# Moving an output copy one step later on ScalarE and the denominators' small term to GpSimd in an attention and expert kernel

## The chip, the cores and the metric
The kernel runs on one core of a Trainium2 chip. The metric is the device time of one execution in microseconds (us). Five engines work beside each other: TensorE (PE, with its weight loads shown as PEld), VectorE (DVE), ScalarE (ACT), GpSimd (POOL) and SyncE (SP, which issues DMAs). They meet through semaphores alone: an instruction increments one when it is done, another waits until it has reached a value.

## The reference
Attention over 2 x 8 heads of 768 positions with 64 dimensions. A query sees only the keys whose six projection signs are the same as its own:

```python
mask = q_bucket[:, :, :, None] == k_bucket[:, :, None, :]
scores = np.where(mask, scale * q @ k.T, -1e9)
scores = scores - np.max(scores, axis=-1, keepdims=True)
attn = np.exp(scores)
attn = attn / (np.sum(attn, axis=-1, keepdims=True) + 1e-09)
attn_out = attn @ v
```

Behind it stand a gated feed-forward layer over the 1536 rows and a layer of 8 experts that sends each row to one of them.

## The kernel before
**Pairs, steps and groups.** The 16 heads are worked as 8 pairs, P = 0 to 7. A pair has 12 steps j; each step takes 128 queries of one head against all 768 keys. Three steps make a group g, so a pair has four groups. A period is one pair's 12 steps. Periods 1 to 4 run in a hardware loop of two passes, the others are written out, with constant semaphore values. Period 8 has no scores of its own and drains what is left, beside the first units of the next layer.

**One step on the engines.** TensorE makes the scores of step j (L941, L942) into one of two banks ps_s. VectorE takes the maximum of each row, negated (L1609). ScalarE takes the exponentials with their sums psums (L1323, an ACTIVATE and a short read of the accumulator). When a group's three steps are done, VectorE adds 1e-9 to the three sums (L1621, denom) and takes the reciprocals (L1623, rden); GpSimd multiplies the three tiles of probabilities by them (L745, the normalization, which also adds alone, a term for rows that see no key, made on GpSimd at L734). The code calls this `denoms(P, g)` on VectorE and `put_alone(P, g)` on GpSimd.

**LAG = 5 steps later** TensorE transposes the normalized tiles, two blocks of keys in a step (L956), ScalarE copies each block to a high part in fp32r (L1333, `highs`), and VectorE subtracts to get the low part (L1629, `lows`). One step after that, TensorE multiplies both parts with v (L971, L973). Once a group's six blocks are summed, ScalarE copies the lower half of the output bank to SBUF (L1338, `half_out`) and VectorE adds the upper half to it (L1635, `x_out`), which frees the bank.

**The order of the work** is written out by hand in each engine's `period`. ScalarE before: highs(j), exps(j), then, at j = 2, 5, 8, 11, half_out. VectorE: max(j), at j = 0, 3, 6, 9 the denominators of the group before, lows(j), at the same j x_out, and at j = 1, 4, 7, 10 a comparison that makes bits for the next pair (L1584, L1586). GpSimd: alone of group g, then the three normalizations of group g, then a slot of other work: splitting q, k and v of later pairs into high and low parts (L630, L634, L650, L671), in periods 5 and 6 also squares for the next layer's norm (L701, L705), in period 7 low parts and weights for that layer (L716, L719, L762). `wait_apart` is GpSimd's wait; inside the loop it also increments a semaphore of its own.

In period 0, j = 3, ScalarE does one of the normalizations itself (L1399). At j = 0 of periods 1 to 5 it scales the queries of a later pair (L1318). In period 7 it makes high parts for the next layer (L1360) at the steps named in HIGHS_BESIDE_EXPS.

**What needs what around the change.** rden needs denom, and lows(j) stands behind rden in VectorE's queue. The normalization of a group needs rden and alone. The transposes of a group need its three normalizations, two steps later. x_out needs half_out.

Of the kernel before, what the change touches and what calls it, by code (L numbers as in the profile page):

```python
# [13 lines left out]
ALU = mybir.AluOpType  # L14
# [4 lines left out]
LAG = 5  # L19
# [7 lines left out]
def wait(eng, sem, value):  # L27

    if isinstance(value, int) and value <= 0:
        return  # L30
    eng.wait_ge(sem, value)


def build(nc, q, k, v, proj, w_gate, w_val, w_out, rms_g, router, out_gate, w1, w2, out):
# [17 lines left out]
    TG = N // G  # L52
    NT = N // P128
    E, _, FE = w1.shape
    CF = FE // P128

# [26 lines left out]
    with ExitStack() as ctx:  # L83
        addr = [nc.sbuf_base + 64]

        def at(name, shape, dt, offset=None):
            size = 4 if dt != BF16 else 2
            for n in shape[1:]:
                size *= n
            if offset is None:  # L90
                offset = addr[0] = (addr[0] + 31) // 32 * 32
                addr[0] += size
            return nc.alloc_sbuf_tensor_at(name, shape, dt, offset=offset)
# [4 lines left out]
        def sem(name):  # L98
            return ctx.enter_context(nc.semaphore(name))
# [81 lines left out]
        psums = at("psums", [P128, PRING], F32)  # L181
        denom = at("denom", [P128, PRING], F32)
# [88 lines left out]
        for i in range(3):  # L271
# [12 lines left out]
        ps_o = psum("ps_o", [P128, 512], F32)  # L284
        ps_p = psum("ps_p", [P128, 512], F32)

        names = ("first_low proj_places q_own proj_in const_set ident_ready proj_split proj_ready proj_ready_second prefilled "
                 "cleared blocks_set blocks_ready scales_ready first_high second_low ahead_high q_scaled qk_high qk_low v_split proj_made bits_ready scores_ready max_done "
                 "alone_put first_norm exp_done denom_done rden_ready norm_done turned high_ready low_ready pv_done "
                 "half_ready x_done pool_passed "  # L290
# [4 lines left out]
                 "hidT_high hidT_low "  # L295
                 "down_made outs_ready").split()
        sems = {n: sem(n) for n in names}
        (first_low, proj_places, q_own, proj_in, const_set, ident_ready, proj_split, proj_ready, proj_ready_second, prefilled, 
         cleared, blocks_set, blocks_ready, scales_ready, first_high, second_low, ahead_high, q_scaled, qk_high, qk_low, v_split, proj_made, bits_ready, scores_ready, max_done,
         alone_put, first_norm, exp_done, denom_done, rden_ready, norm_done, turned, high_ready, low_ready, pv_done,  # L300
         half_ready, x_done, pool_passed,
# [26 lines left out]
        def cols_of(tg):  # L328
            return slice((tg % 2) * G, (tg % 2 + 1) * G)
# [25 lines left out]
        def steps_of(P, j, lag):  # L355

            back = (j - lag) % PAIR_STEPS
            return (P if j >= lag else P - 1), back // 3, back % 3
# [58 lines left out]
        SQUARES_01 = 12  # L417
        LATE_LOWS = {0: slice(0, 2), 1: slice(2, 4), 2: slice(4, 5), 3: slice(5, 6), 4: slice(6, 8)}
        EARLY = {0: 2, 1: 6, 2: 2, 3: 2, 4: 2, 5: 2}
        HIGHS_BESIDE_EXPS = {1: 0, 3: 1, 5: 2, 7: 3, 10: 4}  # L420
        HIGHS_IN_TAIL = {0: (5,), 1: (6, 7)}

        def high_of(tg, c):
# [196 lines left out]
        def _(pool):  # L620
            def wait_apart(sem, value):

                wait(pool, sem, value)
                if not isinstance(value, int):
                    pool.sem_inc(pool_passed, 1)
# [101 lines left out]
            def put_alone(P, g):  # L727
                c = slice(3 * g, 3 * g + 3)

                wait_apart(norm_done, 12 * (P - 1) + 3 * g + 3)  # L730
                wait_apart(max_done, 12 * P + 3 * g + 3)
                if not (isinstance(P, int) and P == 0):
                    pool.wait_ge(first_norm, 1)
                nc.gpsimd.tensor_scalar(alone[:, c], negmax[:, c], MASKED, 1.0 / S,  # L734
                                        ALU.is_ge, ALU.mult).then_inc(alone_put, 1)
                wait_apart(alone_put, 4 * P + g + 1)

            def period(P, slots):
                for g in range(4):
                    put_alone(P, g)  # L740
                    wait_apart(rden_ready, 4 * P + g + 1)
                    own = 2 if isinstance(P, int) and P == g == 0 else 3
                    for j in range(3 * g, 3 * g + own):
                        pr = probs[:, j]
                        nc.gpsimd.tensor_scalar(pr, pr, rden[:, j:j + 1], alone[:, j:j + 1],  # L745
                                                ALU.mult, ALU.add).then_inc(norm_done, 4 - own if j % 3 == 1 else 1)
                    for steps, n in slots[g]:
                        some(n, steps)
# [89 lines left out]
            with pool.Fori(0, 2) as i:  # L838
                P = 2 * i + 1
# [452 lines left out]
        def _(act):  # L1292
# [28 lines left out]
            def exps(P, j):  # L1321
                wait(act, max_done, 12 * P + j + 1)
                nc.scalar.activation(probs[:, j].rearrange("p (a n) -> p a n", a=2), third(ps_s[j % 2]), ACT.Exp,  # L1323
                                     bias=negmax[:, j:j + 1],
                                     accum_out=psums[:, j:j + 1]).then_inc(exp_done, 1)

            def highs(P, g, jj):
                for kt in (2 * jj, 2 * jj + 1):
                    u = 6 * g + kt
                    wait(act, turned, 24 * P + u + 1)  # L1330

                    wait(act, pv_done, 24 * P + u - 3)
                    nc.scalar.activation(pT_h[u % 4][:], ps_t[kt % 2][:, 0:G], ACT.Copy).then_inc(high_ready, 1)  # L1333

            def half_out(P, g):
                wait(act, pv_done, 24 * P + 6 * (g + 1))
                wait(act, x_done, 4 * P + g)
                nc.scalar.activation(o_half[D:2 * D, :], value_banks[g % 2][D:2 * D, 0:G], ACT.Copy).then_inc(half_ready, 1)  # L1338
# [19 lines left out]
            def high_xn(b, c, cols=slice(0, S)):  # L1358

                nc.scalar.activation(xn[:, b, 0, c, cols], xT[:, C * b + c, cols], ACT.Copy,  # L1360
                                     scale=gain[:, c:c + 1]).then_inc(xnh_made, 1)
# [7 lines left out]
            def period(P, par, before=True, s=True, ahead=True):  # L1369
                for j in range(PAIR_STEPS):  # L1370
                    Pt, g, jj = steps_of(P, j, LAG)
                    if (j >= LAG and s) or (j < LAG and before):
                        highs(Pt, g, jj)
                    if s:
                        exps(P, j)
                    Pv, g, jj = steps_of(P, j, LAG + 1)
                    if jj == 2 and ((j >= LAG + 1 and s) or (j < LAG + 1 and before)):
                        half_out(Pv, g)
                    if s and not ahead and j in HIGHS_BESIDE_EXPS:
                        if j == 1:  # L1380
                            act.wait_ge(gates_in, 48)
                            act.wait_ge(scores_ready, PAIR_STEPS * LAST_PAIR)
                        tg, c = divmod(HIGHS_BESIDE_EXPS[j], C)
                        high_xn(0, c, cols_of(tg))
                    if not s and j in HIGHS_IN_TAIL:
                        for n in HIGHS_IN_TAIL[j]:
                            tg, c = divmod(n, C)
                            high_xn(0, c, cols_of(tg))
                    if not s and j in (1, 2, 3):
                        high_xn(1, j - 1)  # L1390
                    if not s and j == 0:
                        root((0, 1))
                    if not s and j == 4:
                        high_last(0)
                    if isinstance(P, int) and P == 0:
                        if j == 3:
                            act.wait_ge(rden_ready, 1)
                            act.wait_ge(alone_put, 1)
                            nc.scalar.activation(probs[:, 2], probs[:, 2], ACT.Identity, bias=alone[:, 2:3],  # L1399
                                                 scale=rden[:, 2:3]).then_inc(first_norm, 1)  # L1400
                        if j in (0, 3, 4):
                            high_ahead(1, 1, max(0, j - 2))
                        if j in (7, 8, 9):
                            high_ahead(2, 0, j - 7)
                    elif j == 0 and (not isinstance(P, int) or P <= LAST_PAIR - 2):
                        scale_queries(P + 2, par)
# [14 lines left out]
            with act.Fori(0, 2) as i:  # L1421
                P = 2 * i + 1
# [157 lines left out]
        def _(dve):  # L1580
# [31 lines left out]
            def denoms(P, g):  # L1612

                n = 4 * P + g + 1
                c = slice(3 * g, 3 * g + 3)

                wait(dve, norm_done, 3 * (n - 4))
                if not (isinstance(P, int) and P == 0):
                    dve.wait_ge(first_norm, 1)
                wait(dve, exp_done, 3 * n)  # L1620
                nc.vector.tensor_scalar(denom[:, c], psums[:, c], 1e-9, None, ALU.add).then_inc(denom_done, 1)  # L1621
                wait(dve, denom_done, n)
                nc.vector.reciprocal(rden[:, c], denom[:, c]).then_inc(rden_ready, 1)  # L1623

            def lows(P, g, jj):
# [122 lines left out]
            with dve.Fori(0, 2) as i:  # L1748
                P = 2 * i + 1
# [286 lines left out]
```

## Time and profile before

| | us |
|---|---|
| median of 3 runs | 757.99 |
| lowest, highest | 757.68, 758.33 |
| the profiled execution's own time | 758.07 |
| its span in the trace | 756.3 |
| TensorE busy | 743.0 (98%) |
| VectorE busy | 477.7 (63%) |
| ScalarE busy | 376.2 (50%) |
| GpSimd busy | 301.3 (40%) |

The profile is of one execution. Times in the trace count from the start of the span; the span is shorter than the execution's own time by what lies around it. The attention runs from about 10 to 254 us of it, the gated layer to 446 us, the rest is routing and experts. Busy shares over the whole span mix these stages. A row of the timeline tells the start, the time, the engine and line, what is written from what, how many instructions are merged in the row, and in brackets how long the engine had been idle before it and what released it.

### The profile page before, as it was taken

Reading aid. Unit: us, or ns where it says so; the run is one execution under the profiler, and the core shown is the slowest. Engines: PE = TensorE matmul, PEld = TensorE weight load, DVE = VectorE, ACT = ScalarE, POOL = GpSimd, SP = SyncE. Lnnn points to the kernel's source line nnn. Section 1 sums busy time; section 2 is a strip of 40 time slices with the busy share of each in tenths; the row PEclk is TensorE's granted clock in tenths of the full one; section 3 lists DMA queues with packets and bytes.
Section 4 is the critical chain, followed back from the end, with each engine's and each line's share of the span. In section 5 each row is a group of like instructions: output and inputs, shape, how many; then the busy total and the mean of one; then the engine's idle time right before and its main releaser. Section 6 shows DMA issues by size and latency. Waiting matters only on the chain.

```text
span 756.3 us, 13441 instructions
## 1 busy us (share of the span) xinstructions
PE 743.0 (98%) x4565; PEld 679.5 (90%) x4565; DVE 477.7 (63%) x928; ACT 376.2 (50%) x675; POOL 301.3 (40%) x348
## 2 busy tenths in 40 slices
PE   8999999999999999999999999999999999999996
PEld 7799899889889999999999998888899998889985
DVE  8999999999998753434443453335376654565430
ACT  5988888888898411111111124443436444455521
POOL 7877777878888664333334100111110111000111
PEclk9999999999999999999999999999999999999999
DMA  7897788678410131211111031004146767866400
GB/s 213 234 277 205 207 235 215 193 193 217 127 33 29 57 98 51 64 52 42 42 42 42 0 127 55 29 29 139 42 158 209 241 189 232 257 219 205 156 25 23
DMA packets 54677, 98.33 MB, mean 130 GB/s; under 512 B 7042, under 2 KB 21390, under 8 KB 54625
## 3 DMA queue, kind: packets, MB, share of 16 engines
q1 hardware_dynamic: 50390, 87.69, 39.5%
q0 software_dynamic: 2240, 6.31, 2.4%
q10 hardware_dynamic: 1995, 3.65, 2.0%
q8 instruction: 30, 0.49, 0.3%
q14 instruction: 22, 0.18, 0.1%
HBM read 57.99 MB, written 22.89 MB: 107 GB/s over the span
## 4 chain that ended last, share of the span: by engine, by line
PE 87%; DVE 8%; issue 2%; ACT 1%; POOL 1%; POOLq 0%; DVEq 0%
PE ps_s L1003 13%; PE ps_t L1162 13%; PE ps_s L1243 8%; PE ps_t L1003 7%; PE ps_t L956 6%; PE ps_p L1273 6%; PE ps_t L1273 6%; PE ps_s L1248 4%; DVE pT_l L1629 3%; PE ps_o L1003 3%; PE ps_p L1003 3%; PE ps_s L941 3%; PE ps_s L942 3%; DVE negmax L1609 3%; PE ps_o L971 2%
## 5 line engine op out<-in xcount | busy, mean ns | idle before, releaser
L745 POOL TENSOR_SCALAR probs<-probs,rden,alone 128x768 f32<-128x768 f32 x95 | 93.0, 991 | 33.5 <-DVE rden L1623 33.2
L1629 DVE TENSOR_TENSOR pT_l<-ps_t,pT_h 128x384 fp32r<-128x384 f32 x192 | 97.5, 549 | 3.4 <-ACT pT_h L1333 2.5
L1003 PE MATMUL ps_s<-xn,w_h 128*128 128x384 f32 x384 | 97.5, 334 | 0.0
L1323 ACT ACTIVATE probs<-ps_s,negmax 128x768 f32<-128x768 f32 x96 | 86.9, 905 | 16.5 <-DVE negmax L1609 16.1
L1609 DVE TENSOR_REDUCE negmax<-ps_s 128x1 f32<-128x770 f32 x96 | 91.1, 948 | 3.1 <-PE ps_s L942 2.5
L1333 ACT ACTIVATE pT_h<-ps_t 128x384 fp32r<-128x384 f32 x192 | 85.0, 490 | 13.9 <-PE ps_t L956 12.6
L956 PE MATMUL ps_t<-ident,probs 128*128 128x128 f32 x576 | 86.7, 281 | 2.7 <-DVE pT_l L1629 1.5
L1797 DVE TENSOR_TENSOR expert_w<-piece,expert_w 128x2048 fp32r<-128x2048 f32 x32 | 72.5, 2288 | 17.3 <-ACT expert_w L1491 17.2
L880 POOL DMA_INDIRECT out_dram<-rows_out,rows_in x16 | 16.0, 1001 | 167.4 <-ACT rows_out L1521 167.4
L956 PEld LDWEIGHTS ps_t<-ident,probs 128*128 128x128 f32 x576 | 63.7, 141 | 20.6 <-DVE pT_l L1629 8.6
L1003 PEld LDWEIGHTS ps_s<-xn,w_h 128*128 128x128 f32 x384 | 69.4, 188 | 0.0
L941 PE MATMUL ps_s<-k_a,q_a 128*128 128x384 f32 x192 | 65.2, 339 | 1.5 <-ACT probs L1323 0.9
L874 POOL DMA_INDIRECT routed<-x,dest x12 | 11.8, 981 | 137.2 <-DVE x L1879 111.4
L942 PE MATMUL ps_s<-k_b,q_b 128*128 128x384 f32 x192 | 64.8, 338 | 0.0
L1003 PE MATMUL ps_s<-xn,w_l 128*128 128x384 f32 x192 | 64.1, 334 | 0.0
L1491 ACT ACTIVATE expert_w<-piece 128x2048 fp32r<-128x2048 f32 x32 | 60.2, 1908 | 0.2 <-issue 0.2
L1243 PE MATMUL ps_s<-rowsT_h,expert_w 128*128 128x240 f32 x448 | 59.6, 275 | 0.0
L1970 DVE SCALAR_TENSOR_TENSOR hidT_l<-ps_s,hidT_h 128x480 fp32r<-128x480 f32 x32 | 20.9, 655 | 60.2 <-ACT hidT_h L1513 60.2
L1162 PE MATMUL ps_t<-wo_h,hs_h 128*128 128x512 f32 (+1 forms) x144 | 57.9, 402 | 0.0
L1243 PEld LDWEIGHTS ps_s<-rowsT_h,expert_w 128*128 128x128 f32 x448 | 55.2, 189 | 0.7
L1162 PE MATMUL ps_t<-wo_h,hs_l 128*128 128x512 f32 (+1 forms) x144 | 55.1, 383 | 0.0
L1162 PE MATMUL ps_t<-wo_l,hs_h 128*128 128x512 f32 (+1 forms) x144 | 54.9, 381 | 0.0
(298 smaller groups left out, 1688.5 us busy)
## 6 DMA issues: line engine op xcount, KB each, us to landing
piece<-in_moe_w_dram SPq DMA_DIRECT2D x32, 1024.0 KB, 6.4
routed<-filler SPq DMA_DIRECT2D x60, 257.0 KB, 4.8
k_a<-qk_h SPq DMA_DIRECT2D x28, 192.0 KB
rows_in<-routed ACTq DMA_DIRECT2D x7, 481.9 KB, 4.6
rawv<-in_v_dram SPq DMA_DIRECT2D x8, 384.0 KB, 6.3
w_raw<-in_moe_w_gate_dram SPq DMA_DIRECT2D x12, 256.0 KB, 3.0
w_raw<-in_moe_w_val_dram SPq DMA_DIRECT2D x12, 256.0 KB, 3.3
wo_raw<-in_moe_w_out_dram SPq DMA_DIRECT2D x12, 256.0 KB, 2.7
```

The lines of the kernel that those rows point to most:

```text
L745: nc.gpsimd.tensor_scalar(pr, pr, rden[:, j:j + 1], alone[:, j:j + 1], ALU.mult, ALU.add).then_inc(norm_done, 4 - own if j % 3 == 1 else 1)
L941: nc.tensor.matmul(o, q_a[par][:, r, queries], k_a[par][:, r, keys], start=True, stop=False)
L942: mm = nc.tensor.matmul(o, q_b[par][:, r, queries], k_b[par][:, r, keys], start=False, stop=True)
L956: mm = nc.tensor.transpose(ps_t[kt % 2][:, i * P128:(i + 1) * P128], probs[:, 3 * g + i, kt * P128:(kt + 1) * P128], ident[:])
L1003: mm = nc.tensor.matmul(unit_banks[tg][w][:, 0:G], a_[par][:, w, c, :], xn_at(tg, part, c), start=(n == 0), stop=(n == 3 * C - 1))
L1162: mm = nc.tensor.matmul(bank, a_[par][:, f, :], b_[:, f, cols], start=(f == 0 and n == 0), stop=(f == NF - 1 and n == 2))
L1243: nc.tensor.matmul(place(f), a_[:, side, c, f * P128:(f + 1) * P128], high[:, c, :], start=(c == 0 and t == 0), stop=False)
L1273: mm = nc.tensor.matmul(out_banks[half][0:HALF], a_[:, c, half_cols(half)], b_[:, side, c, :], start=(c == 0 and t == 0), stop=(c == CF - ...
L1323: nc.scalar.activation(probs[:, j].rearrange("p (a n) -> p a n", a=2), third(ps_s[j % 2]), ACT.Exp, bias=negmax[:, j:j + 1], accum_out=psu ...
L1333: nc.scalar.activation(pT_h[u % 4][:], ps_t[kt % 2][:, 0:G], ACT.Copy).then_inc(high_ready, 1)
L1609: nc.vector.tensor_reduce(negmax[:, c], with_floor(ps_s[j % 2]), AX.XY, ALU.max, negate=True).then_inc(max_done, 1)
L1629: nc.vector.tensor_tensor(pT_l[u % 4][:], ps_t[kt % 2][:, 0:G], pT_h[u % 4][:].bitcast(F32), ALU.subtract).then_inc(low_ready, 1)
```

## The change
A new semaphore, first_denom, serves the first group of the first pair alone, where VectorE still adds the small term itself. For the 31 other groups the addition moves to GpSimd, into `put_alone`, behind alone, and VectorE waits for it before the reciprocals. On ScalarE, half_out moves from behind exps(j) at j = 2, 5, 8, 11 to between highs and exps of the step after. In period 7 one of the high parts for the next layer moves from step 3 to step 2.

```diff
-        HIGHS_BESIDE_EXPS = {1: 0, 3: 1, 5: 2, 7: 3, 10: 4}
+        HIGHS_BESIDE_EXPS = {1: 0, 2: 1, 5: 2, 7: 3, 10: 4}
...
                 nc.gpsimd.tensor_scalar(alone[:, c], negmax[:, c], MASKED, 1.0 / S,
                                         ALU.is_ge, ALU.mult).then_inc(alone_put, 1)
                 wait_apart(alone_put, 4 * P + g + 1)
+                if not (isinstance(P, int) and P == g == 0):
+                    wait_apart(exp_done, 12 * P + 3 * g + 3)
+                    nc.gpsimd.tensor_scalar(denom[:, c], psums[:, c], 1.0, 1e-9, ALU.mult,
+                                            ALU.add).then_inc(denom_done, 1)
...
                     if (j >= LAG and s) or (j < LAG and before):
                         highs(Pt, g, jj)
+                    Pv, g, jj = steps_of(P, j, LAG + 2)
+                    if jj == 2 and ((j >= LAG + 2 and s) or (j < LAG + 2 and before and s) or j == 0 and not s):
+                        half_out(Pv, g)
                     if s:
                         exps(P, j)
                     Pv, g, jj = steps_of(P, j, LAG + 1)
-                    if jj == 2 and ((j >= LAG + 1 and s) or (j < LAG + 1 and before)):
+                    if jj == 2 and j < LAG + 1 and not s:
                         half_out(Pv, g)
...
-                wait(dve, exp_done, 3 * n)
-                nc.vector.tensor_scalar(denom[:, c], psums[:, c], 1e-9, None, ALU.add).then_inc(denom_done, 1)
-                wait(dve, denom_done, n)
+                if isinstance(P, int) and P == g == 0:
+                    dve.wait_ge(exp_done, 3)
+                    nc.vector.tensor_scalar(denom[:, c], psums[:, c], 1e-9, None, ALU.add).then_inc(first_denom, 1)
+                    dve.wait_ge(first_denom, 1)
+                else:
+                    wait(dve, denom_done, n - 1)
                 nc.vector.reciprocal(rden[:, c], denom[:, c]).then_inc(rden_ready, 1)
```

## Rows read from the trace of the kernel before

**Rows 1.** The page: the busy line of part 1, the head of the chain.
```profile
PE 743.0 (98%) x4565; PEld 679.5 (90%) x4565; DVE 477.7 (63%) x928; ACT 376.2 (50%) x675; POOL 301.3 (40%) x348
...
PE 87%; DVE 8%; issue 2%; ACT 1%; POOL 1%; POOLq 0%; DVEq 0%
```

**Rows 2.** Busy time of each engine by stretch; behind PEclk, DMA share and GB/s.
```profile
46.00:186.00 140.00, 140.00 (x896) 126.01 (x895) 137.72 (x259) 121.02 (x264) 109.45 (x141) 1.00 0.79 213
```

**Rows 3.** Waits between 46 and 186 us: total us, times, longest.
```profile
ACT probs L1323 <- DVE negmax L1609: 10.3, 33, 0.5
...
POOL qk_l L650 <- POOL qk_h L671: 2.2, 12, 0.2
```

**Rows 4.** Timeline of VectorE, start of period 4.
```profile
124.89 0.15 DVE L1621 TENSOR_SCALAR denom<-psums 128x3 f32<-128x3 f32 x1
125.08 0.17 DVE L1623 RECIPROCAL rden<-denom 128x3 f32<-128x3 f32 x1
125.25 1.02 DVE L1629 TENSOR_TENSOR pT_l<-ps_t,pT_h 128x384 fp32r<-128x384 f32 x2
...
127.75 1.02 DVE L1629 TENSOR_TENSOR pT_l<-ps_t,pT_h 128x384 fp32r<-128x384 f32 x2
```

**Rows 5.** Timeline of ScalarE, the same stretch.
```profile
124.22 0.48 ACT L1338 ACTIVATE o_half<-ps_p 64x384 f32<-64x384 f32 x1
...
127.09 0.88 ACT L1333 ACTIVATE pT_h<-ps_t 128x384 fp32r<-128x384 f32 x2
```

**Rows 6.** Timeline of GpSimd, one period of the loop.
```profile
104.24 2.93 POOL L745 TENSOR_SCALAR probs<-probs,rden,alone 128x768 f32<-128x768 f32 x3 [0.96 <-DVE rden L1623]
...
111.36 2.92 POOL L745 TENSOR_SCALAR probs<-probs,rden,alone 128x768 f32<-128x768 f32 x3 [1.58 <-DVE rden L1623]
...
118.47 2.92 POOL L745 TENSOR_SCALAR probs<-probs,rden,alone 128x768 f32<-128x768 f32 x3 [1.09 <-DVE rden L1623]
...
125.46 2.92 POOL L745 TENSOR_SCALAR probs<-probs,rden,alone 128x768 f32<-128x768 f32 x3 [1.47 <-DVE rden L1623]
```

**Rows 7.** GpSimd and one transpose of TensorE behind it, periods 5 to 7.
```profile
177.87 0.51 POOL L671 TENSOR_SCALAR qk_h<-raw 128x384 fp32r<-128x384 f32 x1
178.47 1.01 POOL L650 TENSOR_TENSOR qk_l<-raw,qk_h 128x384 fp32r<-128x384 f32 x1
...
209.89 2.93 POOL L745 TENSOR_SCALAR probs<-probs,rden,alone 128x768 f32<-128x768 f32 x3 [1.09 <-DVE rden L1623]
...
212.88 0.87 PE L956 MATMUL ps_t<-ident,probs 128*128 128x128 f32 x6 [0.25 <-POOL probs L745]
```

**Rows 8.** All small additions for alone: ns shortest, median, longest.
```profile
L734 POOL TENSOR_SCALAR alone<-negmax x32: 237/243/282, 17.4 to 238.2; 128x3 f32<-128x3 f32 x32
```

**Rows 9.** Timeline of GpSimd, normalizations from period 5 to the first of period 6.
```profile
167.75 2.91 POOL L745 TENSOR_SCALAR probs<-probs,rden,alone 128x768 f32<-128x768 f32 x3 [0.89 <-DVE rden L1623]
...
174.87 2.92 POOL L745 TENSOR_SCALAR probs<-probs,rden,alone 128x768 f32<-128x768 f32 x3 [0.41 <-DVE rden L1623]
...
181.85 2.93 POOL L745 TENSOR_SCALAR probs<-probs,rden,alone 128x768 f32<-128x768 f32 x3 [0.60 <-DVE rden L1623]
...
188.85 2.93 POOL L745 TENSOR_SCALAR probs<-probs,rden,alone 128x768 f32<-128x768 f32 x3 [0.28 <-DVE rden L1623]
```

**Rows 10.** Timeline of GpSimd and VectorE in period 7.
```profile
216.63 2.92 POOL L745 TENSOR_SCALAR probs<-probs,rden,alone 128x768 f32<-128x768 f32 x3 [0.79 <-DVE rden L1623]
...
223.08 0.24 POOL L734 TENSOR_SCALAR alone<-negmax 128x3 f32<-128x3 f32 x1
223.47 2.90 POOL L745 TENSOR_SCALAR probs<-probs,rden,alone 128x768 f32<-128x768 f32 x3
...
223.70 1.02 DVE L1629 TENSOR_TENSOR pT_l<-ps_t,pT_h 128x384 fp32r<-128x384 f32 x2 [0.41 <-ACT pT_h L1333]
...
238.55 3.32 POOL L745 TENSOR_SCALAR probs<-probs,rden,alone 128x768 f32<-128x768 f32 x3
```

**Rows 11.** Timeline of GpSimd, group 2 of period 0.
```profile
33.17 2.92 POOL L745 TENSOR_SCALAR probs<-probs,rden,alone 128x768 f32<-128x768 f32 x3 [0.35 <-DVE rden L1623]
```

More of the change, by code:

```diff
@@ L285, in build @@
         ps_p = psum("ps_p", [P128, 512], F32)
-        names = ("first_low proj_places q_own proj_in const_set ident_ready proj_split proj_ready proj_ready_second prefilled "
+        names = ("first_denom first_low proj_places q_own proj_in const_set ident_ready proj_split proj_ready proj_ready_second prefilled "
                  "cleared blocks_set blocks_ready scales_ready first_high second_low ahead_high q_scaled qk_high qk_low v_split proj_made bits_ready scores_ready max_done "
@@ L297, in build @@
         sems = {n: sem(n) for n in names}
-        (first_low, proj_places, q_own, proj_in, const_set, ident_ready, proj_split, proj_ready, proj_ready_second, prefilled,
+        (first_denom, first_low, proj_places, q_own, proj_in, const_set, ident_ready, proj_split, proj_ready, proj_ready_second, prefilled,
          cleared, blocks_set, blocks_ready, scales_ready, first_high, second_low, ahead_high, q_scaled, qk_high, qk_low, v_split, proj_made, bits_ready, scores_ready, max_done,
```

## The prediction
> **What bounds the kernel now.** I read the page first. TensorE is 98% busy and VectorE 63% [rows 1], which hides that the stages differ: the change touches the attention alone, so I took busy time by stretch. From 46 to 186 us, the middle of the attention, VectorE works 137.72 of 140 us, 98.4%, with TensorE at its full clock; ScalarE has 19 us to spare and GpSimd 30 [rows 2]. In the list of waits of that stretch VectorE does not stand as a waiter at all, while TensorE's transposes wait for its low parts. So VectorE sets the pace there and TensorE's 100% is overlap of modelled ends. Its timeline shows the queue packed: at a group's end it spends 125.08 - 124.89 = 0.19 us on denom, then goes to the reciprocals and, without a gap, to the low parts [rows 4]. The third reading is GpSimd's timeline, since it gets the work: what counts is its idle time ahead of each group's normalizations, all of it ended by rden [rows 6, 9]. The chain that ended last is TensorE's for 87% of the span [rows 1], from 224 us on nearly without a break, and behind the attention TensorE is packed to the end, so a microsecond saved before should arrive at the end.
>
> **What the change takes away.** Denom leaves VectorE in 31 groups. Where VectorE is the bound, each is worth 0.19 us; 31 x 0.19 = 5.9 us is the ceiling of this part, if nothing else comes to bound.
>
> **ScalarE's copy.** half_out takes 0.48 us and sat ahead of highs. Now highs goes first, so the high part is ready about 0.5 us earlier, which matters because lows would otherwise start 0.19 us earlier and find it barely done. half_out itself ends behind highs, about 0.9 us later; VectorE needs it only behind lows, at 125.25 + 1.02 = 126.27, and at 124.22 + 0.5 + 0.9 = 125.6 it is there: cost nothing, the cover being the pair of low parts. The exponentials behind it start some 0.2 us later, covered by ScalarE's waits for the maximum, 10.3 / 33 = 0.3 us each [rows 3]. The one place without that cover is j = 0 of periods 1 to 5, where the scaling of queries follows: highs(1) at 127.09, one block about 0.44 us, leaves its first part at 127.53 for lows at 127.75 [rows 4, 5]. Late by 0.2 and wanted 0.19 sooner, it costs VectorE about 0.2 us, which eats the 0.19 of that boundary. Period 7's high part, moved by one step, keeps its length and its number: nothing, with ScalarE's slack around it as cover. No DMA is moved, and no queue of SyncE is passed.
>
> **What GpSimd gets.** A small operation of the shape of alone: 0.243 us [rows 8]. But it stands in a closed loop: normalization, slot of other work, alone, wait, denom, VectorE's reciprocal, next normalization. VectorE stops at rden until it comes, with lows, x_out and the next maximum queued behind it, and TensorE and ScalarE behind those. The hop from the end of alone to the next normalization is, in the loop of periods 1 to 4: the wait for its own result, 2.2 / 12 = 0.18 us [rows 3]; a second wait, not in the trace, between nothing and another 0.18, taken as 0.09; the operation, 0.24; its arrival at VectorE, taken from the nearest row, GpSimd to TensorE 212.88 - (209.89 + 2.93) = 0.06 [rows 7]; the reciprocal, 0.17; and its way to GpSimd, 125.46 - 125.25 = 0.21 [rows 4, 6]. Sum 0.95. In the written-out periods the own wait is only 178.47 - (177.87 + 0.51) = 0.09 [rows 7] and I take no second one: 0.78, less some 0.03 for the shorter way: 0.75. The rule for a boundary is then: the idle time in the bracket is what the hop may take. It gives max(-0.19, hop - idle).
>
> **The sum.** Period 0: groups 1 to 3 and the first of period 1 idle 0.91, 0.35, 0.78 and 1.85, the second shown [rows 11]: -0.16 + 0.40 - 0.03 - 0.19 = 0.0. Periods 1 to 4 repeat one pattern, one period of which is shown [rows 6]: 1.58 and 1.47 give -0.19 each, 1.09 gives -0.14, 0.96 gives 0. That is -0.52 a period, -2.1 for the four; the boundary into period 5 gives 0 by ScalarE, above. Period 5, where squares fill GpSimd's slots [rows 9]: 0.89, 0.41, 0.60, 0.28 give -0.14 + 0.34 + 0.15 + 0.47 = +0.8. Period 6: 1.11, 1.15 and 1.09 give -0.19 each, 0.79 gives 0, the last two shown [rows 7, 10]: -0.6. Period 7, first boundary: GpSimd has no idle time, 223.08 + 0.24 to 223.47 is only passage. Its next normalizations come 0.6 late but have time; what counts is lows at 223.70, which waited for ScalarE. New: 223.32 + 0.09 + 0.24 + 0.06 + 0.17 = 223.88, so +0.2 [rows 10]. The rest of period 7 is TensorE's, and its last group lies beside TensorE's early units: between 0 and +0.15, taken as +0.1. Sum: 0 - 2.1 + 0.8 - 0.6 + 0.2 + 0.1 = **-1.6 us**. The execution's own 758.07 becomes 756.5; the median 757.99, 0.08 below it, becomes **756.4 us**. A measurement of this kernel can tell about 0.2%, 1.5 us, from no change, so this sits at that edge.
>
> **Where a page bears on the hop.** Alone lasts 0.24, but from its start to the next start on GpSimd, with nothing else to wait for, it takes 223.47 - 223.08 = 0.39 us [rows 10]. I count passage between instructions. The Trainium skill says the same ("Perfetto Trace Analysis", GPSIMD Engine Instruction): go by start-to-start spacing, as a GpSimd duration in the profile is not reliable. By durations alone the hop would lose 0.27 in the loop and 0.09 outside, and the sum would be about -3.3 us; by spacing it is the -1.6 above.
>
> **Rivals.**
> A. *The hop is short enough.* If it takes 0.2 us less than I think, boundaries at 0.96 and 1.09 gain in full (+0.19 and 0.05, in four periods: 1.0 us less the ScalarE step), and period 5 loses 0.2 instead of 0.8. Total about -3.0 to -3.5: 754.5 to 755. For it: the parts of the hop may overlap. Against: each was taken from a row. Its end, all bounds gone, is -5: 753.
> B. *The gain is given back.* About 16 boundaries go by GpSimd, so the sum is zero once the hop is 0.1 us longer. Also ScalarE or TensorE may hold what VectorE frees: 757.5 to 758.5.
> C. *Slower, by GpSimd.* From 0.1 us up the hop wins, and at +0.3 us the total is -1.6 + 16 x 0.3 = +3.2: 761.2. The place is period 5, with three of four boundaries late already, and the pair of 0.96 and 1.09 in each loop period. One mechanism would be a port: GpSimd's last three normalizations take 3.32 instead of 2.92 us [rows 10], where VectorE runs operations on two SBUF operands, 0.13 us each. Against: beside the attention's VectorE work, alone never took over 0.282 us [rows 8]. The Trainium skill ("Perfetto Trace Analysis", Optimizing Scalar/DVE Operations) warns that the two share a read port, so moving work between them might not help; by that rule with 0.13 us in each hop the sum would be about +0.5. The trace does not show it for this shape.
> D. *It does nothing it says*: exp_done comes so late on ScalarE that GpSimd waits for it. In the rows ScalarE is done with the third exponential at 124.2, VectorE wants the reciprocals at 124.9; 0.2 + 0.24 + 0.06 fits. It would take 0.2 us more to bind, and lands in B.
>
> **How the numbers follow.** Forecast 0.45, spread from -0.8 to -2.6, of which some 0.28 is past 1.5 us; A 0.17, all faster; B and D 0.25, nearly all within; C 0.13, slower by over 1.5 us in nearly all. So faster 0.45, same 0.43, slower 0.12. The range leaves out the far end of A and most of C: 753.9 to 759.4.
>
> **What would show it.** Right: VectorE's list of waits, empty of GpSimd before, shows rden <- GpSimd in period 5 and at two boundaries of each loop period; the loop period shrinks from 28.2 to 27.7 us; period 5 grows by about 0.8; GpSimd's idle time ahead of the normalizations goes to nothing there. Wrong: no such waits, or a loop period of 27.4 (A), or a loop period unchanged with VectorE waiting in three or four boundaries (C), or waits of VectorE for ScalarE's high parts in every group (B).

## The result and the profile after

The changed kernel takes 753.61 us (median of 6 runs, 753.4 to 753.91) against 758.0 (757.68 to 758.5): ratio 0.9944, interval 0.9934 to 0.9954. That is 4.4 us faster, where 1.6 were forecast; it lies just past the low end of the range, 753.9. The profiled execution took 753.91 us, its span is 752.2.

The page of the changed kernel, busy line and head of the chain, against [rows 1]:

```profile
PE 739.0 (98%) x4565; PEld 680.2 (90%) x4565; DVE 469.9 (62%) x897; ACT 377.1 (50%) x675; POOL 306.7 (41%) x379
PE 88%; DVE 4%; POOL 3%; issue 2%; ACT 2%; POOLq 0%; DVEq 0%; ACTq 0%
```

VectorE has 31 instructions fewer and GpSimd 31 more, as the edit says. The chain's share on VectorE fell from 8 to 4% and GpSimd's rose from 1 to 3%. Busy time from 46 to 186 us, columns as in [rows 2]:

```profile
46.00:186.00 140.00, 140.00 (x915) 130.03 (x914) 135.41 (x244) 124.73 (x270) 115.47 (x166) 1.00 0.80 220
```

VectorE is less packed: 135.41 of 140 us, so 4.6 us idle where it had 2.3. The list of waits for the same stretch names most of it (waiter, what it waited for, total us, times, longest):

```profile
DVE pT_l L1639 <- ACT pT_h L1337: 2.0, 4, 0.6
DVE rden L1633 <- POOL denom L739: 1.2, 3, 0.5
POOL denom L739 <- POOL alone L734: 1.1, 4, 0.3
```

Both forecast kinds of wait are here: VectorE for GpSimd's small term, 3 times, all at the boundaries of period 5, and VectorE for a high part, 0.5 us once a period, behind step 0 where ScalarE scales queries. The waits for the small term at two boundaries of each loop period, which the prediction names as a sign, are not there, and a loop period takes 27.5 us, nearer to its rival A (27.4) than to its own 27.7. What was missed stands in VectorE's timeline, a group boundary of the loop, the maximum, the reciprocals and the low parts:

```profile
108.24 0.94 DVE L1616 TENSOR_REDUCE negmax<-ps_s 128x1 f32<-128x770 f32 x1
109.11 0.16 DVE L1633 RECIPROCAL rden<-denom 128x3 f32<-128x3 f32 x1
109.19 0.98 DVE L1639 TENSOR_TENSOR pT_l<-ps_t,pT_h 128x384 fp32r<-128x384 f32 x2
...
125.66 1.02 DVE L1639 TENSOR_TENSOR pT_l<-ps_t,pT_h 128x384 fp32r<-128x384 f32 x2 [0.48 <-ACT pT_h L1337]
```

From the start of the reciprocals to the start of the low parts it takes 109.19 - 109.11 = 0.08 us; before it took 125.25 - 125.08 = 0.17 [rows 4]. With denom's own 0.19 gone the boundary is 0.28 shorter, not 0.19. GpSimd's normalizations show it by group (one period of the loop, then period 5 to the start of 7):

```profile
102.68 2.92 POOL L749 TENSOR_SCALAR probs<-probs,rden,alone 128x768 f32<-128x768 f32 x3 [0.68 <-DVE rden L1633]
...
109.48 2.92 POOL L749 TENSOR_SCALAR probs<-probs,rden,alone 128x768 f32<-128x768 f32 x3 [0.68 <-DVE rden L1633]
...
116.30 2.92 POOL L749 TENSOR_SCALAR probs<-probs,rden,alone 128x768 f32<-128x768 f32 x3 [0.42 <-DVE rden L1633]
...
123.03 2.92 POOL L749 TENSOR_SCALAR probs<-probs,rden,alone 128x768 f32<-128x768 f32 x3 [0.70 <-DVE rden L1633]
...
164.33 2.93 POOL L749 TENSOR_SCALAR probs<-probs,rden,alone 128x768 f32<-128x768 f32 x3 [0.43 <-DVE rden L1633]
...
170.69 0.24 POOL L734 TENSOR_SCALAR alone<-negmax 128x3 f32<-128x3 f32 x1
171.02 0.20 POOL L739 TENSOR_SCALAR denom<-psums 128x3 f32<-128x3 f32 x1
171.64 2.92 POOL L749 TENSOR_SCALAR probs<-probs,rden,alone 128x768 f32<-128x768 f32 x3 [0.42 <-DVE rden L1633]
...
185.92 2.92 POOL L749 TENSOR_SCALAR probs<-probs,rden,alone 128x768 f32<-128x768 f32 x3 [0.41 <-DVE rden L1633]
...
212.52 2.92 POOL L749 TENSOR_SCALAR probs<-probs,rden,alone 128x768 f32<-128x768 f32 x3 [0.41 <-DVE rden L1633]
```

102.68 to 109.48 is 6.80 us, where 104.24 to 111.36 was 7.12 [rows 6]. By stretches between starts of the first normalization, in us:

| stretch | before | after | change | forecast |
|---|---|---|---|---|
| period 0 to first group of 1 | 28.89 | 29.14 | +0.25 | 0.0 |
| periods 1 to 4 | 105.88 | 102.91 | -2.97 | -2.1 |
| into period 5 | 6.95 | 7.01 | +0.06 | 0 |
| period 5 | 28.22 | 28.39 | +0.17 | +0.8 |
| period 6 | 27.78 | 26.60 | -1.18 | -0.6 |
| from period 7 to the end | 539.67 | 539.68 | 0.0 | +0.3 |

The sum is -3.7. Two later traces have the same instructions (e3_highs_back, which differs in period 7 alone, and g2_changed_again, both below). The three repeat the rows from period 1 on to 0.1 us, but period 0 takes 29.14, 28.76 and 29.43 in them, so its +0.25 cannot be told from scatter. The remaining 0.4 of the two traces' difference lies before the first normalization, at 18.91 and 18.47 us; in other profiled executions here, with the same instructions up to it, it comes between 18.3 and 19.0, so no cause in the change is claimed for it.

### The profile page after: what moved, and what is told of

Its sections match the earlier page's. It is cut to its first block, busy times and chain, and to the rows that moved or that the text cites. A ratio compares the mean times of both kernels' runs of the same rounds, so it can differ in the third digit from the quotient of the medians.

```text
span 752.2 us, 13455 instructions
## 1 busy us (share of the span) xinstructions
PE 739.0 (98%) x4565; PEld 680.2 (90%) x4565; DVE 469.9 (62%) x897; ACT 377.1 (50%) x675; POOL 306.7 (41%) x379
## 4 chain that ended last, share of the span: by engine, by line
PE 88%; DVE 4%; POOL 3%; issue 2%; ACT 2%; POOLq 0%; DVEq 0%; ACTq 0%
PE ps_s L1007 13%; PE ps_t L1166 13%; PE ps_s L1247 8%; PE ps_t L960 7%; PE ps_t L1007 7%; PE ps_p L1277 6%; PE ps_t L1277 6%; PE ps_s L1252 4%; PE ps_o L1007 3%; PE ps_p L1007 3%; PE ps_s L945 3%; PE ps_s L946 3%; PE ps_o L975 2%; PE ps_p L975 2%; PE ps_o L977 2%; PE ps_p L977 2%
## 5 line engine op out<-in xcount | busy, mean ns | idle before, releaser
L960 PE MATMUL ps_t<-ident,probs 128*128 128x128 f32 x576 | 83.3, 278 | 2.5 <-DVE pT_l L1639 1.6
L960 PEld LDWEIGHTS ps_t<-ident,probs 128*128 128x128 f32 x576 | 65.8, 141 | 15.3 <-DVE pT_l L1639 6.0
```

The source lines that it names most:

```text
L960: mm = nc.tensor.transpose(ps_t[kt % 2][:, i * P128:(i + 1) * P128], probs[:, 3 * g + i, kt * P128:(kt + 1) * P128], ident[:])
```

## The experiments

**Theory H** was formed on the gap of 0.17 against 0.08: before, the low parts at a group's start did not wait for VectorE's queue but for ScalarE's high part, which stood behind the output copy. **Theory V** is the prediction's: VectorE's own queue was the bound there. Two kernels take the halves of the change apart.

The copy alone, on the kernel before:

```diff
                         highs(Pt, g, jj)
+                    Pv, g, jj = steps_of(P, j, LAG + 2)
+                    if jj == 2 and (...as in the change...):
+                        half_out(Pv, g)
                     if s:
                         exps(P, j)
...
-                    if jj == 2 and ((j >= LAG + 1 and s) or (j < LAG + 1 and before)):
+                    if jj == 2 and j < LAG + 1 and not s:
```

> The kernel before with only the output copy moved between high parts and exponentials; the small term stays on VectorE. Theory H: before the change the low parts at a group's start waited for ScalarE's high part, which stood behind the copy, and started 0.18 us after the reciprocals instead of 0.09. Then the copy's move alone is worth 0.09 us in some 25 groups, about 2 us, less up to 0.5 us where the query scaling follows: 756 to 757 us, and the low parts start 0.09 us after the reciprocals start. Theory V, that of the prediction: VectorE's queue alone was the bound there, and the copy's move by itself is worth nothing: 757.7 to 758.5 us.

It took 756.0 us, ratio 0.9976 (0.9965 to 0.9986). VectorE's timeline of this kernel:

```profile
110.66 0.15 DVE L1624 TENSOR_SCALAR denom<-psums 128x3 f32<-128x3 f32 x1
110.84 0.18 DVE L1626 RECIPROCAL rden<-denom 128x3 f32<-128x3 f32 x1
110.94 1.02 DVE L1632 TENSOR_TENSOR pT_l<-ps_t,pT_h 128x384 fp32r<-128x384 f32 x2
...
127.63 1.02 DVE L1632 TENSOR_TENSOR pT_l<-ps_t,pT_h 128x384 fp32r<-128x384 f32 x2 [0.27 <-ACT pT_h L1333]
```

The low parts start 0.10 us after the start of the reciprocals, not 0.17: the 0.07 to 0.08 that was hidden is gone with denom still there, and a group shrinks from 7.12 to 7.04. By stretches it gains 0.41 us in periods 1 to 4, 0.46 in period 5, 0.35 in period 6 and 0.48 from there to the end. The gain is what H says, and V's "nothing" is out.

The small term alone (the changed kernel with the copy and the high part of period 7 back in their old places):

```diff
-                    Pv, g, jj = steps_of(P, j, LAG + 2)
-                    if jj == 2 and (...as in the change...):
-                        half_out(Pv, g)
...
-                    if jj == 2 and j < LAG + 1 and not s:
+                    if jj == 2 and ((j >= LAG + 1 and s) or (j < LAG + 1 and before)):
                         half_out(Pv, g)
```

> The changed kernel with the output copy back behind the exponentials and the high part of period 7 back in step 3; the small term stays on GpSimd. Theory H: the low parts still wait for the high part behind the copy, so in the loop's periods nothing is won (a group stays near 7.1 us), and period 5 pays its 0.8 us for GpSimd: 758 to 759.5 us. Theory V: 0.19 us per group as in the prediction's sum, about 756.4 us.

It took 757.27 us, ratio 0.9994 (0.9985 to 1.0003): no change that can be told. Its VectorE, and one line of its waits from 46 to 186 us:

```profile
109.83 0.16 DVE L1630 RECIPROCAL rden<-denom 128x3 f32<-128x3 f32 x1
110.20 1.02 DVE L1636 TENSOR_TENSOR pT_l<-ps_t,pT_h 128x384 fp32r<-128x384 f32 x2 [0.21 <-ACT pT_h L1337]
```

```profile
DVE pT_l L1636 <- ACT pT_h L1337: 3.7, 18, 0.2
```

Denom's 0.19 us has become a wait of 0.21 us for the high part, 18 times in this stretch, and the groups are 7.12 and 7.00 us as before. H's core holds. Its size for the whole was wrong: I expected 758 to 759.5 for period 5, which did lose 0.54 us, but period 6 gained 0.45, and period 0 was 0.54 shorter, which is within the scatter of that period.

So in the loop (periods 1 to 4, 105.88 us before) the copy alone gives 0.41, the small term alone 0.0, both 2.97 us. The first opens room that only the second can use, and the other way round.

The high part of period 7 back in step 3, in the changed kernel (`{1: 0, 3: 1, 5: 2, 7: 3, 10: 4}`):

> The changed kernel with the high part for the next layer back in step 3 of period 7. Theory: this part costs and wins nothing, within 0.3 us of the changed kernel (753.6). Rival: ScalarE's order copy, exponentials, high part in step 3 delays the high parts of step 4 in period 7, once, by up to 0.5 us: 754.1.

754.05 us, ratio 0.9948 (0.9934 to 0.9962), its span 752.2 as the changed kernel's. No difference can be told from noise, which fits the price of nothing.

**The hop through GpSimd.** One more operation in it:

```diff
                     wait_apart(exp_done, 12 * P + 3 * g + 3)
+                    nc.gpsimd.tensor_scalar(spare[:], psums[:, c], 1.0, 1e-9, ALU.mult, ALU.add)
                     nc.gpsimd.tensor_scalar(denom[:, c], psums[:, c], 1.0, 1e-9, ALU.mult,
```

> The changed kernel with one more small operation on GpSimd (into a tile that nothing reads) between the wait for the exponentials and the small term: the hop grows by one passage, about 0.25 to 0.3 us. By the prediction's rule 16 boundaries go by GpSimd, each pays all of it: +4 us or more, 757.5 to 758.5. If instead the boundaries of the loop have 0.2 to 0.3 us to spare between the small term and the reciprocals, as the trace of after suggests, only the late ones of periods 5 to 7 pay, five to seven of them: +1 to +2 us, 754.8 to 755.8.

757.87 us, ratio 1.0001 (0.9992 to 1.001): 4.2 us above the changed kernel, the total that the prediction's count of 16 boundaries gives (16 x 0.26 = 4.2), and not the 1 to 2 us that I had by then read from the trace. GpSimd at one boundary of it:

```profile
117.07 0.20 POOL L740 TENSOR_SCALAR spare<-psums 128x3 f32<-128x3 f32 x1 [0.29 <-POOL alone L735]
117.33 0.20 POOL L741 TENSOR_SCALAR denom<-psums 128x3 f32<-128x3 f32 x1
117.95 2.94 POOL L751 TENSOR_SCALAR probs<-probs,rden,alone 128x768 f32<-128x768 f32 x3 [0.42 <-DVE rden L1635]
```

The start-to-start step is 0.26 us for an operation of 0.20. In the loop a period grows from 27.49 to 27.90, 0.2 to 0.3 of it at this one boundary and 0.1 at the one behind the scaling of queries. The two traces differ by 1.6 us in periods 1 to 4 and the boundary into 5, 1.05 in period 5, 0.9 in period 6 and 0.1 behind it; the last 0.5 lies before the first normalization, where the two kernels have the same instructions. By the prediction's rule it would be about 2.1 in the loop (8 boundaries) and 0.3 in period 6 (one), so the match of the total is in part luck. Here the whole gain of the change is given back: the change stands 0.26 us per group from being worth nothing.

**Three edits for the three waits of after.** First, GpSimd's wait for its own result behind the small term:

```diff
-                wait_apart(alone_put, 4 * P + g + 1)
                 if not (isinstance(P, int) and P == g == 0):
                     wait_apart(exp_done, 12 * P + 3 * g + 3)
                     nc.gpsimd.tensor_scalar(denom[:, c], ...).then_inc(denom_done, 1)
+                wait_apart(alone_put, 4 * P + g + 1)
```

> The changed kernel with GpSimd's wait for its own result alone moved from ahead of the small term to behind it, so the hop from alone to the reciprocals loses what that wait takes, 0.09 us in the written-out periods and up to 0.29 in the loop. If boundaries that go by GpSimd pay the hop one for one, as the longer hop did in the other direction (+0.26 us of hop gave +4.2), some 10 to 16 of them give back 0.1 us each: 752.0 to 752.8. Rival: the passage between the two operations stays, since GpSimd only starts the second when the first is done: within 0.3 of the changed kernel, 753.6.

754.52 us, 0.9953 (0.994 to 0.9967): 0.9 us slower than the changed kernel, against both expectations. GpSimd in period 5 of this kernel:

```profile
171.09 0.25 POOL L734 TENSOR_SCALAR alone<-negmax 128x3 f32<-128x3 f32 x1
171.42 0.20 POOL L738 TENSOR_SCALAR denom<-psums 128x3 f32<-128x3 f32 x1
172.10 2.94 POOL L749 TENSOR_SCALAR probs<-probs,rden,alone 128x768 f32<-128x768 f32 x3 [0.49 <-DVE rden L1633]
```

Here, in written-out code, it is 0.33 us from alone to denom with or without the wait between them. From denom to the normalization it is 0.68 instead of 0.62, with two waits ahead of it in place of one. In the loop the gap ahead of the term did go at one boundary a period (0.53 to 0.32 us from alone to denom), but that boundary did not hold VectorE. The hop got longer by 0.06 where it is paid: period 5 grows by 0.34 us and period 6 by 0.27. The 0.3 that periods 1 to 4 lose is spread over their boundaries and not explained.

Second, the scaling of queries one step later:

```diff
-                    elif j == 0 and (not isinstance(P, int) or P <= LAST_PAIR - 2):
+                    elif j == 1 and (not isinstance(P, int) or P <= LAST_PAIR - 2):
                         scale_queries(P + 2, par)
```

> The changed kernel with ScalarE's scaling of queries in periods 1 to 5 at step 1 instead of step 0. In the trace of after, VectorE waits 0.48 us for the high part behind that scaling once a period. Theory: at step 1 it falls where ScalarE waits 0.55 us for a transpose and costs 0 to 0.2, so five periods give back 0.2 to 0.45 each: 751.5 to 752.6. Rival: it only moves the wait by a step: 753.3 to 753.9.

752.11 us, 0.9923 (0.9909 to 0.9936): 1.5 us below the changed kernel, as the theory says. VectorE of this kernel at step 0 of period 4:

```profile
121.76 0.17 DVE L1633 RECIPROCAL rden<-denom 128x3 f32<-128x3 f32 x1
121.84 0.99 DVE L1639 TENSOR_TENSOR pT_l<-ps_t,pT_h 128x384 fp32r<-128x384 f32 x2
...
124.31 1.02 DVE L1639 TENSOR_TENSOR pT_l<-ps_t,pT_h 128x384 fp32r<-128x384 f32 x2
```

The low parts of step 1, with 0.48 us of waiting in after, start without a gap.

Third, the small term back on VectorE in the five groups that waited longest for it: ON_VECTOR = ((0, 0), (5, 2), (5, 3), (6, 0), (7, 1), (7, 3)) takes the place of the one exception in both engines' code.

> The changed kernel with the small term back on VectorE in the five groups where the trace of after shows VectorE waiting for GpSimd's term: groups 2 and 3 of period 5, 0 of 6, 1 and 3 of 7 (0.41, 0.21, 0.55, 0.51, 0.96 us). Each wait is exchanged for 0.19 us of VectorE and the 0.33 us of GpSimd goes: 0.2 + 0.0 + 0.4 + 0.3 give back about 0.9, the last lies beside TensorE: 752.5 to 753.0. If GpSimd's loop itself is the bound there, more comes back, up to 1.5. Rival: what VectorE saves is held by ScalarE or TensorE in those groups: 753.6.

752.55 us, 0.9928 (0.9915 to 0.9942): 1.1 us below the changed kernel. Period 5 takes 27.65 us where it took 28.39, from period 7 to the end it is 539.23 where it was 539.68, and VectorE's waits for GpSimd are gone from its list.

All three, and then the two that gained:

> The three edits together. If they act at different boundaries (loop, first step of a period, periods 5 to 7) their gains add: 749.8 to 751.5. If one bound covers the others, no better than the best of the three alone.

751.02 us, 0.9911 (0.9896 to 0.9926).

> The changed kernel with the scaling at step 1 and the five late small terms on VectorE, and GpSimd's own wait where the change has it. The two edits gave 1.5 and 1.1 us by themselves and act at different boundaries: 751.0. The wait behind the small term cost 0.9 us by itself, because each normalization then starts 0.06 us later behind its reciprocals; in the kernel with all three (751.0) it should cost a part of that: 750.2 to 751.0. Rival: the three together were already at the next bound, TensorE: 751.0 exactly as before.

751.01 us, 0.9912 (0.9898 to 0.9925): the same, which the theory (a part of the 0.9 us comes back) and its rival (TensorE is the next bound) both allowed. The traces bear out neither. With all three edits the wait behind the term gains in the loop and costs in period 6: periods 1 to 4 take 101.95 us against 102.41 here, period 6 26.78 against 26.52. At the boundary behind the scaling, the last maximum and the reciprocals, first with the two edits, then with all three:

```profile
100.36 0.96 DVE L1626 TENSOR_REDUCE negmax<-ps_s 128x1 f32<-128x770 f32 x1
101.38 0.17 DVE L1643 RECIPROCAL rden<-denom 128x3 f32<-128x3 f32 x1
...
100.00 0.96 DVE L1626 TENSOR_REDUCE negmax<-ps_s 128x1 f32<-128x770 f32 x1
100.88 0.17 DVE L1643 RECIPROCAL rden<-denom 128x3 f32<-128x3 f32 x1
```

From start to start it is 1.02 us and 0.88. At most boundaries of both kernels it is 0.87. So with the two edits VectorE waits some 0.14 us for GpSimd's term at this boundary, again without idle time in any list. Busy time from 46 to 186 us of this kernel:

```profile
46.00:186.00 140.00, 140.00 (x925) 131.87 (x925) 138.05 (x249) 124.59 (x272) 117.19 (x165) 1.00 0.80 221
```

VectorE is at 98.6% again, now with 31 - 5 = 26 operations fewer. It is nearly the bound by its own work, but the 0.14 us a period above is still a wait.

> The changed kernel itself once more, as the measure for the others on the same chip: 753.4 to 754.1.

753.67 us, 0.9946 (0.9932 to 0.9959), as the first time; g1 is 2.7 us below it, beside it on the same chip.

## Why the prediction was right and wrong

**Wrong: the term of 0.19 us a group, and the copy at nothing.** The prediction has "each is worth 0.19 us" and the queue going from the reciprocals to the low parts "without a gap". The rows it rests on show the reason against it: the reciprocals end at 125.08 + 0.17 = 125.25 and the low parts start there [rows 4], though VectorE overlaps such neighbours by 0.08 when nothing holds it (after, 109.11 + 0.16 against 109.19). ScalarE's high parts of that step, before:

```profile
124.73 0.87 ACT L1333 ACTIVATE pT_h<-ps_t 128x384 fp32r<-128x384 f32 x2
```

The first of the two blocks was done at 124.73 + 0.44 = 125.17, and the low parts started 0.08 us behind it. It was a wait of 0.08 us that shows no idle time, so no list of waits had it, and its absence from that list was taken as proof that VectorE was the bound. Measured, the boundary is 0.28 to 0.32 us shorter: 0.19 from the term and 0.09 from the copy. The prediction did see that the low parts, 0.19 us sooner, would find the high part "barely done" without the copy's move. The second experiment shows that it would not be done at all: they wait 0.21 us, and the term alone buys nothing in the loop. This step makes about half of the miss of 2.8 us: periods 1 to 4 and 6 gained 4.15 us where 2.7 were forecast. The next largest part is the 0.6 us of period 5, below.

The same comparison finds one more such place, in both kernels: one step behind a group's start the low parts begin 0.97 us after the start of the maximum (119.79 to 120.76 before, 117.54 to 118.51 after), at the other steps 0.86. No run here shows what holds them.

**Right in kind, off in size: the scaling of queries.** Forecast as eating 0.2 us at step 0 of periods 1 to 5, it leaves VectorE waiting 0.48; the boundary is 7.12 where 7.0 was expected, and the same wait (0.55 at period 1) makes the boundary into period 1 7.32 us long where it was 6.96. The last maximum of the group before and the high parts that the wait is for, before and then after:

```profile
124.02 0.94 DVE L1609 TENSOR_REDUCE negmax<-ps_s 128x1 f32<-128x770 f32 x1
127.09 0.88 ACT L1333 ACTIVATE pT_h<-ps_t 128x384 fp32r<-128x384 f32 x2
...
121.78 0.96 DVE L1616 TENSOR_REDUCE negmax<-ps_s 128x1 f32<-128x770 f32 x1
125.14 0.86 ACT L1337 ACTIVATE pT_h<-ps_t 128x384 fp32r<-128x384 f32 x2
```

From the start of that maximum the first block is done after 127.53 - 124.02 = 3.51 us before and 125.57 - 121.78 = 3.79 after: 0.28 later, where 0.2 was taken. VectorE wants it 0.28 sooner, not 0.19, and needs 0.09 us from its end to its own start, which the sum had at nothing. Against the 0.22 us of slack before that makes 0.43, near the 0.48 measured.

**Right in straight code, wrong in the loop: the hop through GpSimd.** The hop in the written-out periods was put at 0.75 us; in after it is 171.64 - 170.93 = 0.71, made of 0.09 (own wait), 0.20 (the term), 0.13 (its way to VectorE), 0.18 (reciprocals) and 0.11 (the way back). The total held better than its parts: 0.06 was said for the way there and 0.18 for the way back. In the loop 0.95 was said, and 116.30 - 115.39 = 0.91 is measured. The rule that the idle time ahead of the normalization is what the hop may take picked out period 5; the three late boundaries changed by +0.19, -0.02 and +0.32, each about 0.15 less than forecast. Of this 0.04 is the hop; about 0.1 is that GpSimd got from a normalization to the work behind it in 2.88 us instead of 3.01, or through the slot that much quicker, with the same instructions. Why was not tried. Wrong was that the hop would hold VectorE in the loop: from the start of the last maximum to the reciprocals it takes 0.86 to 0.88 us at every boundary of periods 1 to 4, so nothing there waited for GpSimd.

**Right: start-to-start spacing.** The Trainium skill ("Perfetto Trace Analysis", GPSIMD Engine Instruction) asks for spacing in place of durations, and the trace agrees: the added operation of 0.20 us cost 0.26 from start to start. The sum by durations, -3.3, would have been nearer to the result, but by the wrong term.

**Rivals.** A came nearest in size, not in mechanism: the hop was as long as thought. B is what the small term does without the copy's move: ScalarE holds what VectorE frees, 757.27 us. C's port did not show: all 31 small terms took 0.196 to 0.200 us, and the last normalizations, beside operations on two SBUF operands, again took longer than the rest (3.60 us for three). D showed in part: GpSimd's term waited for the exponentials 13 times in the stretch from 46 to 186 us, 5.8 us in all, without holding VectorE in the loop (the 0.87 us above).

## What to carry to other kernels

An operation that starts exactly where the one before it ends, on an engine that elsewhere overlaps the two by 0.08 us, may be waiting for somebody, as here: compare the gaps of the same pair of instructions at several places before calling an engine the bound, since a list of waits shows only idle time. When two edits each free a different engine of one closed chain, run both halves; here they gave 0.4 and 0.0 us in the loop apart and 3.0 together. A tiny operation moved to an idle engine costs its whole hop if that engine's next large work waits for the answer, so put it there only where the idle time ahead of that work is longer than the hop: taking it back in the five groups where it was not gained 1.1 us.

## What the runs showed of the hardware

A wait for GpSimd's own result that is already met is not always free: moved behind the small term, ahead of the normalization, it made that start 0.06 to 0.07 us later in periods 5 to 7 (0.68 against 0.62 from the term's start), while in its old place there it cost nothing, 0.33 us between the two starts with it and without. In the loop it was the other way round: nothing ahead of the normalization (0.38 us from the reciprocals' start in both kernels), but 0.53 against 0.32 us from alone to the term where no exponential was waited for. One more small operation of 0.20 us takes 0.26 us from start to start. VectorE starts the next operation 0.08 us ahead of the profiled end of the reciprocals when that one's input is there in time (109.11 + 0.16 against 109.19), and at their end when it is not (125.08 + 0.17 against 125.25).
